# TensorE's attention written as a loop over four chunks, with the products with v as one pass of 64x64 quads

## The reference

```python
# attention: batch 4, 8 heads, 768 tokens, head dim 48
for t in range(S):
    kt, vt, rt = (k[:, :, t], v[:, :, t], r[:, :, t])
    cur = np.einsum('bhd,bhe->bhde', u[None] * kt, vt)
    y[:, :, t] = np.einsum('bhd,bhde->bhe', rt, state + cur)
    state = w[None, :, :, None] * state + np.einsum('bhd,bhe->bhde', kt, vt)
# experts: 3072 tokens of width 384, 8 experts, hidden width 1024
expert_idx = np.argmax(x @ w_gate, axis=1)
out[mask] = gate_w[mask, None] * (np.maximum(x[mask] @ w1[e], 0.0) @ w2[e])
# dense: hidden width 2048, leaky relu 0.01
h = x @ w_in
return np.maximum(0.01 * h, h) @ w_out
```

## Time and profile before

| what | value |
|---|---|
| median of 3 runs | 831.3 us (830.53 to 842.6) |
| profiled execution, its own time | 825.21 us |
| its span | 823.5 us |
| attention's 24 steps in the trace | 13.64 to 148.25 us |
| start of the expert stage's matmuls | 174 us |
| PE, DVE, ACT, POOL busy over the span | 94%, 41%, 26%, 41% |
| mean granted TensorE clock | 0.97 |

### The profile page before, as it was taken

The page is one execution under the profiler, slowest core; times in us unless marked ns, Lnnn a source line. Parts: engine busy times, 40 slices in busy tenths (PEclk is TensorE's granted clock), DMA queues, the critical chain, the costliest instruction groups (busy, mean ns, idle before and its releaser), DMA issues.

```text
span 823.5 us, 17748 instructions
## 1 busy us (share of the span) xinstructions
PE 771.5 (94%) x7200; PEld 707.7 (86%) x7200; DVE 335.7 (41%) x658; ACT 215.1 (26%) x436; POOL 335.3 (41%) x338
## 2 busy tenths in 40 slices
PE   9889889469998989999899999999999999999995
PEld 8778777459998989999889889989988998998994
DVE  7868755613233133223544333433433433433332
ACT  2224433311122112111122232222232223232221
POOL 6568855637767677976991010010010001001001
PEclk9999989779999999999999999999999999999998
DMA  4757654354665355356430000010000000001000
GB/s 145 225 159 208 182 164 148 117 125 136 109 124 150 91 146 157 103 146 146 115 117 1 1 38 1 1 39 1 1 38 0 0 0 38 0 0 39 1 1 39
DMA packets 42611, 66.91 MB, mean 81 GB/s; under 512 B 11413, under 2 KB 31797, under 8 KB 42549
## 3 DMA queue, kind: packets, MB, share of 16 engines
q1 hardware_dynamic: 28944, 50.76, 22.6%
q10 hardware_dynamic: 10533, 5.80, 3.7%
q0 software_dynamic: 3072, 9.45, 3.1%
HBM read 51.42 MB, written 14.59 MB: 80 GB/s over the span
## 4 chain that ended last, share of the span: by engine, by line
PE 79%; POOL 9%; issue 5%; DMA 3%; DVE 2%; ACT 0%; ACTq 0%; POOLq 0%; SPq 0%; DVEq 0%
PE bank L1174 24%; PE bank L1153 24%; PE bank L1114 7%; PE bank L1098 7%; POOL w_lo L134 5%; PE ps_y L833 3%; POOL w_hi L130 2%; DMA stage<-in_moe_w 2%; PE ps_y L818 2%; PE ps_x L790 2%; PE ps_s L770 2%; PE ps_x L786 2%; PE ps_l L854 1%; PE ps_x L845 1%; PE ps_m L804 1%
## 5 line engine op out<-in xcount | busy, mean ns | idle before, releaser
L1042 POOL DMA_INDIRECT out_rows<-rows,ids_i x24 | 23.1, 962 | 358.7 <-ACT rows L1253 353.2
L1318 DVE TENSOR_TENSOR h_lo<-gf,h_hi 128x512 fp32r<-128x512 f32 x96 | 70.2, 732 | 227.4 <-ACT h_hi L1244 227.4
L134 POOL TENSOR_TENSOR w_lo<-stage,w_hi 128x768 fp32r<-128x768 f32 (+1 forms) x70 | 146.4, 2092 | 5.8
L1174 PE MATMUL bank<-w_hi,h_hi 128*128 128x384 f32 x384 | 130.4, 339 | 0.0
L1174 PE MATMUL bank<-w_lo,h_hi 128*128 128x384 f32 x384 | 129.3, 337 | 0.0
L1174 PE MATMUL bank<-w_hi,h_lo 128*128 128x384 f32 x384 | 129.1, 336 | 0.0
L1240 ACT ACTIVATE hc<-bank 128x512 f32<-128x512 f32 x96 | 57.4, 597 | 273.1 <-PE bank L1153 273.1
L1153 PE MATMUL bank<-x_hi,w_hi 128*128 128x512 f32 x288 | 114.0, 396 | 2.3 <-DVE x_lo L1300 2.3
L1153 PE MATMUL bank<-x_lo,w_hi 128*128 128x512 f32 x288 | 114.3, 397 | 0.0
L1153 PE MATMUL bank<-x_hi,w_lo 128*128 128x512 f32 x288 | 113.9, 395 | 0.0
L1281 DVE SCALAR_TENSOR_TENSOR h_lo<-bank,h_hi 128x416 fp32r<-128x416 f32 x64 | 37.7, 591 | 149.5 <-ACT h_hi L1220 149.5
(11 more groups left out here) (170 smaller groups left out, 1185.5 us busy)
## 6 DMA issues: line engine op xcount, KB each, us to landing
stage<-in_moe_w SPq DMA_DIRECT2D x24, 512.0 KB, 6.0
stage<-in_moe_w SPq DMA_DIRECT2D x32, 384.0 KB, 3.1
rows<-x_rows ACTq DMA_DIRECT2D x9, 625.6 KB
x_rows<-pad_row SPq DMA_DIRECT2D x32, 156.4 KB
k_u<-in_k SPq DMA_DIRECT2D x48, 96.0 KB, 3.0
r_u<-in_r SPq DMA_DIRECT2D x48, 96.0 KB, 2.7
v_u<-in_v SPq DMA_DIRECT2D x24, 192.0 KB, 3.5
stage<-in_moe_w_in SPq DMA_DIRECT2D x6, 512.0 KB, 4.3
```

Source lines behind the costliest of these rows:

```text
L134: i = eng.tensor_tensor(w_lo[:, buf, off:off + cols], stage[:, h, 0:cols], w_hi[:, buf, off:off + cols].bitcast(F32), ALU.subtract)
L1174: i = pe.matmul(ps_o[t][:, 0:D], x[:, f % NB, t * P:(t + 1) * P], ww[:, 1, o:o + D], start=f == 0 and x is h_hi and ww is w_hi, stop=f == ...
L1318: dve.tensor_tensor(h_lo[:, f % NB, :], gf[:, f % 2, :], h_hi[:, f % NB, :].bitcast(F32), ALU.subtract).then_inc(gl_ok, 1)
```

## The change

Five things are changed together.

1. TensorE's steps for chunks 1 to 4 are one loop over c; chunks 0 and 5 stay written out. Waits in it compare with a register, and a `waited` increment follows some of them.
2. So that every chunk's code reads the same addresses: RB is 4 instead of 5 (buffers by pair q), x_st has 2 slots instead of 4 (the second half's `state` then waits for `from_state` of the same unit, f_mm), ruk has 4 slots.
3. `scores` writes head 1 into the swapped partition half, v comes three times from HBM (head 0, head 1, and head 1 with its two token halves swapped), and `within` is one pass of 16 products over all four pairs of row half and column half. It waits for `from_state` (f_mm).
4. The transposes are by column slice d and all four batches, from a copy `yr` that ACT makes, at fixed steps; the logits are at pairs 1 and 2, behind `from_state`.
5. SP issues k of unit g+5 after `k_rows` of g+1, r of unit g+4 after `within` of g, v of g+4 after that. DVE forms ruk (`scale`) ahead of the second `state`, and scales r (`scale_r`) right behind it, both ahead of routing. POOL's `scaled_k` waits for the scaled r and for v.

```diff
-            RB = 5
+            RB = HP
+            VC = 3 * B * DH
...
-            x_st = sb("x_st", [P, HP, 4, B * DH + L - DH], stack=st1)
+            x_st = sb("x_st", [P, HP, 2, B * DH + L - DH], stack=st1)
...
+                sp.wait_ge(ka_mm, 1)
+                load_k(RB)
                 for g in range(UN):
+                    if g + 1 + RB < UN:
+                        sp.wait_ge(ka_mm, g + 2)
+                        load_k(g + 1 + RB)
                     if g + RB < UN:
                         sp.wait_ge(y_mm, g + 1)
+                        load_r(g + RB)
                         sp.wait_ge(own_ok, g + 1)
-                        load(g + RB)
+                        load_v(g + RB)
...
-                    pool.wait_ge(ruk_ok, g + 1)
+                    pool.wait_ge(r_ok, g + 1)
+                    pool.wait_ge(v_in[i], g // RB * 16 + 16)
...
                     if j == 1:
                         dve.wait_ge(v_ok, 2 * g + 1)
+                        dve.wait_ge(f_mm, g + 1)
...
+                    for n in due(g):
+                        scale(n)
                     if c < C - 1:
                         state(g, 1)
+                    for n in due(g):
+                        scale_r(n)
                     routing(routed(c, q))
-                    for n in due(g):
-                        scale(n)
...
+                def within(n, q):
+                    pe.wait_ge(f_mm, n + 1)
+                    carried(n)
                     for b in range(B):
                         for j in range(2):
+                            for t in range(2):
+                                ins = pe.matmul(ps_y[halves[j], t, b * L:(b + 1) * L], am[halves[j ^ t], q % 2, t, b, :],
+                                                v_cols(q, j ^ t, 2 * t, b, L), start=False, stop=True,
+                                                skip_group_check=True)
+                    ins.then_inc(y_mm, 1)
...
+                for q in range(HP):
+                    step(0, q)
+                pe.wait_ge(wg_in, 16)
+                with pe.Fori(1, C - 1) as c:
+                    for q in range(HP):
+                        step(c, q)
+                for q in range(HP):
+                    step(C - 1, q)
...
+    thrice = lambda a: np.concatenate([a, np.roll(a[:, :, :, 1:], P // 2, axis=2)], axis=3)
```

More of the change, by code:

```diff
@@ L769, in scores @@
                             for t in range(2):
-                                ins = pe.matmul(ps_s[halves[j], t, b * L:(b + 1) * L], k_u[heads[t], i, b, halves[j]],
-                                                r_u[heads[t], i, b, halves[j]], start=True, stop=True)
+                                ins = pe.matmul(ps_s[halves[j ^ t], t, b * L:(b + 1) * L], k_u[heads[t], q, b, halves[j]],
+                                                r_u[heads[t], q, b, halves[j]], start=True, stop=True)
@@ L801, in update @@
                     for b in range(B):
[L802 removed]
+                        for j in range(1 if last else 2):
                             for t in range(2):
                                 ins = pe.matmul(ps_m[heads[t], j, b * DH:(b + 1) * DH],
[L805 removed]
+                                                km[halves[j], b, heads[t]], v_cols(q, j, t, b, DH),
@@ L863, in ranks, with step @@
                     pe.matmul(ps_tot, ones[:, :], oh[:, :, :], start=True, stop=True).then_inc(rank_mm, 1)
-                pe.wait_ge(warm_ok, 1)
-                for _ in range(WARM):
-                    pe.matmul(ps_s[:, 0, 0:P], ones[:, :], ones[:, :], start=True, stop=True)
-                scores(0)
-                pe.wait_ge(consts, 3)
-                k_rows(0)
-                for _ in range(4):
-                    pe.matmul(ps_y[:, 0, 0:P], ones[:, :], ones[:, :], start=True, stop=True)
-                update(0)
-                for g in range(UN):
-                    c, q = divmod(g, HP)
-                    at = (c - 1) * B + 2 * q
-                    if g + 1 < UN:
-                        scores(g + 1)
-                    if g == HP:
-                        pe.wait_ge(wg_in, 16)
-                    if g == UN - 1:
+                def step(c, q):
+                    n = c * HP + q
+                    first, last = not in_loop(c) and c == 0, not in_loop(c) and c == C - 1
+                    more = not last or q < HP - 1
+                    to_last = last or (not in_loop(c) and n + 1 == (C - 1) * HP)
+                    if more:
+                        scores(n + 1, (q + 1) % HP)
+                    else:
                         pe.wait_ge(y_out, UN - 1)
@@ L910, in on_tensor @@
-                    within(g, True)
-                    if g + 1 < UN:
-                        update(g + 1)
-                    if c > 0 and q < 2:
-                        pe.wait_ge(yt_out, at + 1)
-                        logits(c, 2 * q)
-                        tile(c, 2 * q + 1, ps_x)
+                    if more:
+                        if q == 2 or (first and q < 2):
+                            k_rows(n + 1, (q + 1) % HP, None)
+                        else:
+                            k_rows(n + 1, (q + 1) % HP, c * DC + {3: 1, 0: -1, 1: 0}[q])
@@ new lines, in step @@
+                    from_state(n, q, last)
+                    if not first and q == 1:
+                        logits(c, 0)
+                        logits(c, 1)
+                    if not first and q == 2:
+                        logits(c, 2)
+                        logits(c, 3)
+                    if not first and q == 3:
+                        ranks(c)
+                    within(n, q)
+                    if q == 0 and not first:
+                        tile(n, 2, c * DC)
+                    if q >= 2 and not last:
+                        tile(n, q - 2, c * DC + (q - 1))
@@ new lines, in step @@
+                    if more:
+                        update(n + 1, (q + 1) % HP, to_last)
+                pe.wait_ge(warm_ok, 1)
+                for _ in range(WARM):
+                    pe.matmul(ps_s[:, 0, 0:P], ones[:, :], ones[:, :], start=True, stop=True)
+                scores(0, 0)
+                pe.wait_ge(consts, 3)
+                k_rows(0, 0, None)
+                for _ in range(4):
+                    pe.matmul(ps_y[:, 0, 0:P], ones[:, :], ones[:, :], start=True, stop=True)
```

188 lines of the change are left out of this document (92 added, 96 removed).

## The result

| | before | after |
|---|---|---|
| median, the same chip | 831.5 us | 846.6 us (842.8 to 851.5, 4 runs) |
| ratio, with its 95% interval | | 1.0149, 1.0089 to 1.0209 |
| profiled execution, its own time / span | 825.2 / 823.5 us | 848.7 / 846.9 us |
| start of the expert stage's matmuls | 174 us | 204 us |
| mean granted TensorE clock | 0.97 | 0.93 |

The prediction was 812 us, 799 to 827. The changed kernel is slower, not faster. A ratio is taken over each kernel's runs within 1.5% of its own fastest. (The two medians alone stand 1.8% apart; one of the four runs before took 842.6 us.) Two later comparisons gave 1.0074 and 1.0155, and the kernel before against itself 1.0055 (its interval 1.0027 to 1.0083), so a ratio here is good to some 0.006 to 0.008, whatever its interval says. After is slower by about 1%.

What follows compares the result with a forecast made beforehand. TensorE was taken as the bound, with gaps from late code and lost clock. Chunks 2 to 4 (-11.9), 1 (-3.4), 0 and 5 (-3.8) gave -19.1 us: 825.2 to 806 profiled, median 812, range 799 to 827.

Steps and rivals of the forecast that it cites:

- Part 1: TensorE's loop, chunks 1 to 4: body kept, turns 2 to 4 without code fetches, their 6.6 us of idle gone.
- Rival C: TensorE's loop body isn't kept: chunks 2 to 4 take 66.4 us instead of 57.9; 820 us, chance 0.12.
- Part 2: `within` on all four quads: 0.6 us saved a step, TensorE's work per chunk from 20.1 to 17.7 us.
- F: The quads in `within` gain nothing, as row tiles can't access one PSUM bank simultaneously; 823 us, chance 0.15.
- Part 3: Other engines in attention: VectorE's work unchanged at 17.5 us a chunk, GpSimd's 17.0, level with TensorE's 17.7.
- Part 4: Attention's two-step cycle through r's load, issued when `within` ends: 16.4 to 21.0 us a chunk, taken near 16.4.
- E: The cycle through r's load in attention binds, at 21.0 us a chunk; 818 us, chance 0.11.
- The clock: TensorE's clock in the loop: at 1.00, so 2.6 us of lost clock in chunks 2 to 4 go.
- Rival D: TensorE waits for r and state in nearly every loop step, clock stays at 1.2 GHz; 853 us, chance 0.07.
- The sum: Attention's savings of 11.9, 3.4 and 3.8 us make 19.1; everything behind attention moves with its end.

Runs made afterwards that it cites:

- after_again: The changed kernel, unaltered, traced again on the same chip as before_again; ratio 1.0155 to the kernel before.
- before_again: The kernel before, unaltered, run as if it were a change; ratio 1.0055 to itself.
- unroll: The changed kernel with TensorE's loop written out, nothing else; ratio 1.0133 to the kernel before.
- loop_alone: raw_r_sp with `scores` and `within` as before the change (two passes, no quads), v still loaded three times; ratio 0.9989 to the kernel before.
- filler: The changed kernel with 28 products of ones ahead of `update` of unit 4, where TensorE stood for r; ratio 1.0180 to the kernel before.
- raw_r_sp: sp_order with r loaded into two buffers of its own and scaled into four others, so r is loaded earlier; ratio 0.9960 to the kernel before.
- sp_order: The changed kernel with SP's queue reordered so that nothing ahead of r waits for GpSimd; ratio 0.9977 to the kernel before.
- quads_alone: The kernel before with the quads and v three times, without the loop or new order; ratio 1.019 (two runs, no interval) to the kernel before.
- lodve: raw_r_sp with attention's weight splits moved off GpSimd: w_hi to ScalarE, w_lo to VectorE one step later; ratio 0.9913 to the kernel before.
- route_first: raw_r_sp with w_hi roundings on ScalarE and VectorE's routing ahead of the scaling of r; ratio 0.9953 to the kernel before.
- half_within: The kernel before with 7 of 8 products of the second pass of `within` left out; ratio 1.0807 to the kernel before.
- control: The changed kernel, unaltered, on another chip; ratio 1.0074 to the kernel before.

## Why the prediction was wrong

**Part 1, the loop: right in mechanism.** The body was kept: but for two packets early in turn 2 no code of TensorE came in turns 2 to 4, and its waits for issue in attention were 0.7 us (after_again) against 14.2 (before_again). Rival C falls. But it is worth nothing here (unroll): the gaps that went were replaced by waits for VectorE.

**Part 2, the quads: right in size.** 0.56 us a step, forecast 0.6; F falls. Two row halves wrote one bank in 0.63 us for the 16 products. The rule of the Trainium skill, TensorEngine Tiling (Array Packing), Gotcha 1: PSUM Pressure, that different row tiles cannot access the same bank simultaneously, cost nothing that this trace shows. But 14 us less work on TensorE became 4.3 us in loop_alone, because TensorE doesn't bound this order.

**Part 3, the other engines: the term that was mis-sized.** DVE's "work is unchanged" took durations of before, where routing stood ahead of the scaling, which alone met GpSimd. In the new order what comes behind it meets GpSimd: measured 20 us in chunks 2 to 4 for 17.5. I had read the earlier trace rows as GpSimd held up by VectorE and drew only the gain from it; the hold works the other way too, on several short operations behind the scaling: in the first trace after, the conversion for row_i has a mean of 1370 ns for 169 before.

**Part 4, r one unit later: the step that failed.** It said that r of unit g+4 "is issued when `within` of g ends". It is not: SP's queue is in order and stood 9.5 us at L368 and up to 5.4 at L116 for GpSimd, and VectorE then waited up to 5.6 us for r. I had priced the queue's issues, 0.42 to 1.53 us, and not its waits. The kernel before stands there too (9.7 us at L116 and 4.4 for wg in before_again), but with RB = 5 nobody was waiting for r. E's cycle binds where the queue stands, not at 21.0 us throughout.

**The clock.** Forecast 1.00 in the loop, found 0.60 to 0.92 in the chunks of the loop in the changed kernel's three traces. Rival D had this mechanism at 0.07: waits of over 1.3 us, the lower clock behind them, which stretches TensorE's work so that it rests less but doesn't catch up. It needs no wait in each step, as D had it: with two long ones (4.2 and 3.7 us) and some shorter, a third to half of attention was at the lower level. What exactly makes the clock fall is open (filler). D's 853 was near the 846.6, partly by luck: in the two other comparisons the loss was 6 and 13 us.

**The sum.** Everything behind attention did move with its end, to within 0.3 us in the pair of one chip (642.3 and 642.6 us from the first expert matmul to the end). But that stretch isn't fixed: the kernel before took 649.4 us for it in its first trace, and the seven traces with r in buffers of their own took 645.8 to 655.3, several with waits of TensorE for GpSimd's weight splits. This is where raw_r_sp's earlier end went (attention 9.1 us shorter than sp_order's, the span 1.8 longer). Since the kernel before alone varies by 7 us there, nothing shows that the buffers have to do with it; why it varies is open.

## What to carry to other kernels

Before a load is moved closer to its use, walk its DMA queue: every wait ahead of it in the queue is now a wait of the load. When TensorE's work is cut to the level of VectorE and GpSimd, take their durations from where they overlap in the new order, not from the old means. Don't forecast full clock where TensorE will wait: here it fell in or behind waits of 3.7 and 4.2 us, and the time at the lower level cost up to 12 us more than before. The quads, with the loop, ended clearly below the kernel before only once the loads came in time and GpSimd left VectorE alone, and then by less than 1%.

## What was not expected of the hardware

- VectorE held by GpSimd for 3.40 us on 128x4 elements, over three GpSimd instructions.
- The same instructions at the same times to 0.01 us on two chips, and the clock fell 7 us apart.
- Steps with less work on TensorE didn't get their code faster: 20 packets in chunks 1 to 4 took 97.1 us in quads_alone and 93.3 in before_again, and the waits for issue were longer.
- Signals came late in some traces. In the first trace of the changed kernel VectorE goes on at 99.57, 1.8 us after the scores it waited for had ended:

```profile
96.63 1.14 PE L826 MATMUL ps_s<-r_u,k_u 48*64 48x64 f32 x32
```

```profile
99.57 0.69 DVE L554 TENSOR_TENSOR am<-ps_s,mask_l 128x512 f32<-128x512 f32 x1 [2.02 <-remote]
```

Where no instruction ended close enough to a signal, the profile names the releaser "remote". Such waits add up to 10.0 us in the attention of the first trace (4 of them), and to 7.0, 11.1, 11.4 and 3.2 in filler, lodve, route_first and half_within, which shared one chip; the other thirteen traces have none. They come about where GpSimd scatters rows. They fit attention being 158 us in the first trace and 142 in control and after_again, but they don't carry the loss, since after_again has none and 1.0155. What delays them wasn't tried.
